# First three dense passes split over the columns of chunks 0 to 2 and chunk 3, and the check of w's range moved to GpSimd and ScalarE

## What is computed

```python
for t in range(S):
    cur = np.einsum('bhd,bhe->bhde', u[None] * kt, vt)
    y[:, :, t] = np.einsum('bhd,bhde->bhe', rt, state + cur)
    state = w[None, :, :, None] * state + np.einsum('bhd,bhe->bhde', kt, vt)
x = attention_out.transpose(0, 2, 1, 3).reshape(B * S, H * D)
x = (x @ w_a * (x @ w_b)) @ w_out
h = x @ w_in
out = (h * np.clip(h + 3.0, 0.0, 6.0) / 6.0) @ w_out2
```

## Time and profile before

| | |
|---|---|
| median of 3 runs | 919.12 us (918.99 to 919.4) |
| the profiled execution | 919.12 us |
| its span in the trace | 917.3 us |
| TensorE busy (PE) | 911.9 us |
| VectorE busy (DVE) | 369.5 us |
| ScalarE busy (ACT) | 329.5 us |
| GpSimd busy (POOL) | 184.3 us |

### The profile page before, as it was taken

One profiled execution on the slowest core, in us unless ns is written; L12 is line 12 of the kernel. 1 busy time (PEld: TensorE's weight loads), 2 busy tenths in 40 slices (PEclk: granted clock), 3 DMA queues, 4 the chain that ended last, 5 costly groups with the idle time before them and its releaser, 6 DMA issues.

```text
span 917.3 us, 15108 instructions
## 1 busy us (share of the span) xinstructions
PE 911.9 (99%) x6400; PEld 746.4 (81%) x6400; DVE 369.5 (40%) x607; ACT 329.5 (36%) x651; POOL 184.3 (20%) x168
## 2 busy tenths in 40 slices
PE   8999999999999999999999999999999999999998
PEld 6788888888888888888888888888888888888887
DVE  7746344525443343334222343343343343343332
ACT  6645323232333233242221343433333333333333
POOL 5976102111111111010755570000000000000000
PEclk9999999999999999999999999999999999999999
DMA  8653211121120121131311210100200100100000
GB/s 307 198 167 108 90 50 62 55 90 56 56 110 34 56 110 55 38 129 48 115 50 55 78 50 1 65 5 1 69 1 0 70 1 7 64 0 1 35 1 36
DMA packets 24281, 57.84 MB, mean 63 GB/s; under 512 B 2320, under 2 KB 8080, under 8 KB 24208
## 3 DMA queue, kind: packets, MB, share of 16 engines
q1 hardware_dynamic: 19808, 48.18, 15.6%
q10 hardware_dynamic: 4400, 8.65, 2.5%
HBM read 47.39 MB, written 9.44 MB: 62 GB/s over the span
## 4 chain that ended last, share of the span: by engine, by line
PE 98%; DVE 1%; DMA 0%; ACT 0%; issue 0%; SPq 0%; DVEq 0%; ACTq 0%
PE up_ps L722 32%; PE up_ps L799 21%; PE acc_ps L736 16%; PE acc_ps L813 11%; PE att_ps L813 11%; PE att_ps L614 2%; PE att_ps L677 1%; PE att_ps L682 1%; PE att_ps L646 1%; PE att_ps L663 1%; PE att_ps L671 1%; DMA first_rk<-in_rk_turned 0%; ACT A L854 0%; DVE first_rk L1044 0%; DVE first_A L1067 0%
## 5 line engine op out<-in xcount | busy, mean ns | idle before, releaser
L722 PE MATMUL up_ps<-x_cut,w_up 128*128 128x512 f32 x1296 | 307.3, 391 | 0.2 <-ACT x_cut L867 0.2
L722 PEld LDWEIGHTS up_ps<-x_cut,w_up 128*128 128x128 f32 x1296 | 241.7, 188 | 52.9 <-issue 3.0
L926 ACT ACTIVATE g_cut<-tmp 128x512 fp32r<-128x512 f32 x168 | 106.2, 632 | 214.4 <-DVE tmp L1149 141.6
L1157 DVE SCALAR_TENSOR_TENSOR g_cut<-tmp,g_cut 128x512 fp32r<-128x512 f32 x168 | 125.2, 745 | 117.5 <-ACT g_cut L926 117.5
L736 PE MATMUL acc_ps<-g_cut,w_down 128*128 128x512 f32 x648 | 157.3, 390 | 0.0
L736 PEld LDWEIGHTS acc_ps<-g_cut,w_down 128*128 128x128 f32 x648 | 121.3, 188 | 26.0 <-issue 0.6
L1151 DVE SCALAR_TENSOR_TENSOR tmp<-tmp,up_ps 128x512 f32<-128x512 f32 x96 | 66.1, 689 | 182.9 <-ACT tmp L920 182.9
L920 ACT ACTIVATE tmp<-up_ps,three 128x512 f32<-128x512 f32 x96 | 66.2, 690 | 171.0 <-PE up_ps L799 171.0
L1149 DVE TENSOR_TENSOR tmp<-tmp,up_ps 128x512 f32<-128x512 f32 x72 | 49.5, 688 | 169.7 <-PE up_ps L722 169.6
L799 PE MATMUL up_ps<-x_cut,w_up 128*128 128x512 f32 x432 | 105.7, 389 | 0.0
L799 PE MATMUL up_ps<-x_cut,w_in_first 128*128 128x512 f32 x432 | 105.4, 389 | 0.0
(11 more groups left out here) (109 smaller groups left out, 557.2 us busy)
## 6 DMA issues: line engine op xcount, KB each, us to landing
nat<-in_natural SPq DMA_DIRECT2D x20, 704.0 KB, 6.0
rkT<-in_rk_turned SPq DMA_DIRECT2D x20, 512.0 KB, 3.6
w_raw<-in_moe_w_out SPq DMA_DIRECT2D x28, 192.0 KB, 2.4
layer_out_T<-stage ACTq DMA_DIRECT2D x6, 768.0 KB, 3.4
x_cut<-layer_out_T SPq DMA_DIRECT2D x6, 768.0 KB, 4.3
outT<-stage ACTq DMA_DIRECT2D x5, 768.0 KB, 3.3
w_raw<-in_moe_w_in SPq DMA_DIRECT2D x12, 256.0 KB, 4.6
first_rk<-in_rk_turned SPq DMA_DIRECT2D x4, 512.0 KB, 5.6
```

The lines of the kernel that those rows point to most:

```text
L722: mm = pe.matmul(up_ps[:, m, :], w_up[i // PB][:, a, m, c, cols], x_cut[:, t % 2, b, c, :], start=(z == 0), stop=(z == len(order) - 1))
L926: nc.scalar.activation(g_cut[:, n % GR, HI, :], tmp[:, n % 2, :], ACT.Copy, scale=1.0 if n < TILES * N1 else 1.0 / 6.0).then_inc(s_gh, 1)
L1157: dve.scalar_tensor_tensor(out=lo, in0=tmp[:, n % 2, :], scalar=1.0 if n < TILES * N1 else 1.0 / 6.0, in1=hi.bitcast(F32), op0=ALU.mult, o ...
```

## The change

Five edits. The check of w moves from VectorE to GpSimd (`find_in_range`: two comparisons and a product, put between the fourth and the fifth of the eight masks that GpSimd makes), and the flag is made by one ScalarE instruction, Relu(count + `all_but_one`), straight from PSUM into the integer tile. The count goes into a bank of `att_ps`, not of `acc_ps`. TensorE now waits for three steps of `s_guard`. The dummy behind the count has 1 block, not 2. At the end of `first_chunks` the dummy of 1 block gives way to `first_passes`: the three high-by-high passes of the first `up1`, made over the 384 columns of chunks 0 to 2 as soon as those are there, and again over chunk 3's 128 columns. The first `up1` has six passes left.

```diff
+        def find_in_range(pool):
+            pool.wait_ge(s_w_u, 16)
+            nc.gpsimd.tensor_scalar(in_range[0:W2], w_col[0:W2], W_MIN, None, ALU.is_ge).then_inc(s_guard, 1)
+            nc.gpsimd.tensor_scalar(not_above[0:W2], w_col[0:W2], W_MAX, None, ALU.is_le).then_inc(s_guard, 1)
+            pool.wait_ge(s_guard, 2)
+            nc.gpsimd.tensor_tensor(out=in_range[0:W2], in0=in_range[0:W2], in1=not_above[0:W2],
+                                    op=ALU.mult).then_inc(s_guard, 1)
...
             keep_where(P + MID, every, 1, -1, 0, 1, ALU.is_equal)
+            find_in_range(pool)
             keep_where(2 * P, low_half, 1, -1, 0, 1, ALU.is_gt)
...
             if n == 0 and m == 0:
-                order.sort(key=lambda x: x[2])
+                order = sorted((x for x in order if x[1:] != (HI, HI)), key=lambda x: x[2])
             for z, (c, a, b) in enumerate(order):
-                if n == 0 and m == 0 and z == 2 * KC:
+                if n == 0 and m == 0 and z == KC:
                     pe.wait_ge(s_x_cut, B)
...
+        def first_passes(pe):
+            for chunks in (range(B - 1), range(B - 1, B)):
+                pe.wait_ge(s_x_high, chunks[-1] + 1)
+                if chunks[0] == 0:
+                    pe.wait_ge(s_w_high, KC)
+                cols = slice(chunks[0] * CH, (chunks[-1] + 1) * CH)
+                for c in range(KC):
+                    pe.matmul(up_ps[:, 0, cols], w_up[0][:, HI, 0, c, 0:P], x_cut[:, 0, HI, c, cols],
+                              start=(chunks[0] == 0 and c == 0), stop=False, skip_group_check=True)
...
             outputs(pe, 3)
-            keep_warm(pe, 1)
+            first_passes(pe)
...
-            dve.tensor_scalar(in_range[0:W2], w_col[0:W2], W_MIN, None, ALU.is_ge).then_inc(s_guard, 1)
-            dve.wait_ge(s_guard, 1)
-            dve.scalar_tensor_tensor(out=in_range[0:W2], in0=w_col[0:W2], scalar=W_MAX, in1=in_range[0:W2],
-                                     op0=ALU.is_le, op1=ALU.mult).then_inc(s_guard, 1)
...
-            dve.wait_ge(s_count, 1)
-            dve.tensor_scalar(all_in[:], count_ps, 3.0 * W2 * NP - 1.0, None, ALU.is_ge).then_inc(s_guard, 1)
-            dve.wait_ge(s_guard, 3)
-            dve.tensor_copy(flag[:], all_in[:]).then_inc(s_flag, 1)
...
                 nc.scalar.activation(first_use[:], three[:], ACT.Copy)
+                act.wait_ge(s_count, 1)
+                nc.scalar.activation(flag[:], count_ps, ACT.Relu, bias=all_but_one[:, 0:1]).then_inc(s_flag, 1)
                 flag_act = decide(act)
...
-                pe.wait_ge(s_guard, 2)
+                pe.wait_ge(s_guard, 3)
...
                 keep_warm(pe, 4)
-                keep_warm(pe, 2)
+                keep_warm(pe, 1)
                 first_chunks(pe)
```

More of the change, by code:

```diff
@@ L109, in build @@
             in_range = sb("in_range", [P, NP], of=setup)
-            all_in = sb("all_in", [1, 1], of=setup)
+            not_above = sb("not_above", [P, NP], of=setup)
+            all_but_one = sb("all_but_one", [1, 1], of=setup)
             inv_fine = sb("inv_fine", [P, NP, FINE + 1], of=setup)
@@ L306, in x_view @@
             return x_cut[:, tile % 2, z, :, cols_of(q)]
-        count_ps = acc_ps[0:1, 1, 0:1]
+        count_ps = att_ps[0:1, 0, 0:1]
         HD = H * D
@@ L722, in up1 @@
                 mm = pe.matmul(up_ps[:, m, :], w_up[i // PB][:, a, m, c, cols], x_cut[:, t % 2, b, c, :],
-                               start=(z == 0), stop=(z == len(order) - 1))
+                               start=(z == 0 and n + m > 0), stop=(z == len(order) - 1),
+                               skip_group_check=(n + m == 0))
             mm.then_inc(s_ua if m == 0 else s_ub, 1)
@@ L1182, in vector_layer2, with tables_of_powers @@
                         x2_low(dve, t + 1)
-        def guard_and_tables(dve):
+        def tables_of_powers(dve):
             links = [0]
@@ L1268, in _ @@
                 nc.gpsimd.memset(three[:], 3.0).then_inc(s_three, 1)
+                nc.gpsimd.memset(all_but_one[:], 1.0 - 3.0 * W2 * NP).then_inc(s_three, 1)
                 make_masks(pool)
@@ L1277, in _ @@
             def _(act):
-                act.wait_ge(s_three, 1)
+                act.wait_ge(s_three, 2)
                 nc.scalar.activation(first_use[:], three[:], ACT.Copy)
+                act.wait_ge(s_count, 1)
+                nc.scalar.activation(flag[:], count_ps, ACT.Relu, bias=all_but_one[:, 0:1]).then_inc(s_flag, 1)
                 flag_act = decide(act)
@@ L1301, in _ @@
             def _(dve):
-                guard_and_tables(dve)
+                tables_of_powers(dve)
                 flag_dve = decide(dve)
```

## The result

The changed kernel takes 921.76 us in the median of 9 runs (919.2 to 924.93); the kernel before took 919.4 us in the runs beside it (918.95 to 919.88). The ratio is 1.0033, with a 95% interval of 1.0023 to 1.0042: 0.33% slower. The forecast was 918.7 us and no difference. As telling as the median is the spread: 0.9 us before, 5.7 us after. One run took 919.2, the others form clumps at 921.1 to 921.8 and 923.8 to 924.9.

The account below looks back on a forecast made before the run. TensorE's queue from 20.55 us bounds the kernel, its start set by the front and the hand-over. 917.3 - 0.46 = 916.8 span, plus 1.8 around it, gives 918.66, forecast 918.7 us; range 918.1 to 919.5.

Parts of the forecast that it names:

- The check of w: Step on the start: `in_range` at 3.25 us, 0.28 later than before, covered by 0.3; taken as 0.
- 0.3 us of cover: Ahead of the own weights: 0.1 us of room behind the dummies plus about 0.2 from the halved dummy.
- TensorE's rate rises later: Rival, chance 0.06: gap ahead of the count and smaller dummy delay the rise past 7 us; 918.8 to 919.7.
- the 6.1 that the prediction named as a sign of being wrong: Sign at the start: prediction wrong if TensorE's own weights start later than 6.1 us; expected at 5.97.
- The hand-over: Stretch from 20.55 us to the transposes: they would start at 22.30, not 22.76, a gain of 0.46 us.
- The wide passes: Three 384-column passes in the last dummy's place: 0.63 us from 19.88, ending at 20.51, before the wait ends at 20.55.
- the narrow ones: Three 128-column passes behind chunk 3's high part: 0.34 us with the first load.
- the transposes' 0.08: Time taken for each narrow pass, from the spacing of four 112-column transposes with 128-column weight loads.
- the first load: Extra time of the first narrow pass at the hand-over, its weights loaded behind the wait: 0.10 us.
- The six full passes: Six 512-column passes left in the first `up1`, behind the narrow ones: 0.235 us each, 1.41 together.
- The rule that I set beside it: Skill's load cost at the hand-over: some 107 ns per 128 columns; narrow passes 0.32 instead of 0.24, gain 0.38.
- the margin at piece 19: Narrowest place found later on, piece 19's low part at 48.46 us: margin of 1.1 us shrinks to 0.65, stays open.

Follow-up runs that it names:

- the passes alone: Kernel before with `first_passes` in place of the last dummy and nothing else: 919.27 us, ratio 0.9999.
- the gap filled: Changed kernel plus one more dummy block ahead of the count, in the time TensorE waited for `in_range`: 918.95 us, then 918.97 us when timed again.

## Why the prediction was wrong, point by point

**The step that failed** is in "The check of w": the wait ahead of the count and the halved dummy were charged against 0.3 us of cover and put at 0. What they set off is the rival "TensorE's rate rises later": its mechanism was on the list, at a chance of 0.06 and with the wrong size. It named both causes, and the runs show each to be enough alone: 4 of 6 and 9 of 12 high with the gap, 8 of 12 with the block less, 0 of 11 and 1 of 12 with the gap filled. The price was put at up to 1 us (918.8 to 919.7), from one pair of dummies and one chunk's weights. Chunk 0's mask copy alone is 1.46 us late, and chunk 3's high part 5.35, because the half rate doesn't end with chunk 0: it lasted to some 19 us, and every chunk's own weights and weights are on the path while it does (VectorE and ScalarE, which set the pace before, wait for TensorE). In the two profiles of the levels between, at 921.71 and 920.61, the rise is at about 10 us.

**"Hidden, so nothing"** was the reasoning that let it pass. The gap and the shorter dummy were weighed as work that something else covers; but what the dummies do here, by the runs above, is to bring the rate up, and that was priced only as a rival. The Trainium skill ("TensorE: Matmul & The Clock Gate", section "What's actually happening") says that the engine's clock is throttled by default and activity lifts it, and that the moment isn't tied to the kernel's start. The traces agree, in that records take about twice their time until some moment that differs between executions with the same dummies (about 5.3 us in the profile of before, after 6.1 in that of the passes alone). The same page (section "Seeing it yourself") warns that the trace's own events of this clock have been unreliable. The granted clock here reads 1.00, the 2.4 GHz level, over stretches at half rate. That this half rate is the throttled clock is therefore argued, from the durations and from what sets it off, and no column here shows it.

**The check's lateness.** Forecast 3.25 us for `in_range`; it is 3.46. Each operation takes 0.20 to 0.24 us, as estimated, but they follow each other at 0.31, even the second, which waits for nothing. The count starts at 3.61 and not near 3.4, so the gap was 0.41 us where I had 0.3. The own weights start at 6.17 instead of 5.97: 0.2 late, which I had at 0, and above the 6.1 that the prediction named as a sign of being wrong.

**The hand-over.** Forecast 0.46 us, measured 0.37. The wide passes fit as forecast: they start at 25.24, and the narrow ones wait for chunk 3's high part and not for them. The three narrow weight loads stand from 25.91 to 26.32, 188 ns each, which spaces them by 0.11 us; I took the transposes' 0.08. The transposes were a poor stand-in: their weight loads are recorded at 138 to 143 ns, those of the narrow passes at 186 to 192. Yet the step from the first narrow load to the first full pass is 0.38, forecast 0.34, so that only about 0.05 of it is left for the first load, which I had at 0.10. The six full passes take 1.45 against 1.41, 0.04 more as well. Together that is the 0.09 by which the gain was overrated.

The rule that I set beside it (the Trainium skill, same page, section "LDWEIGHTS (loading the stationary operand)") is that a load costs by its columns, some 107 ns. The measured spacing of 0.11 us agrees. That its gain of 0.38 is also nearly the measured 0.37 is in part luck, since two smaller misses, the first load and the full passes, cancel.

**VectorE, ScalarE, SyncE.** The flag is there at 4.23 us instead of 4.47, the product starts at 5.05 instead of 5.23, since the transfer landed a little earlier in this execution. None of it shows in the time, as forecast. No new wait opened behind 22 us, so the margin at piece 19 held; the 0.6 us for `first_A` at 24.2 is the wait that stood at 18.9 before, with 0.5.

## What to carry to other kernels

Dummy matmuls that keep an engine busy are not slack, and a wait put ahead of them is not free even if nobody waits for their results. Where early records show the engine at half rate, price a shorter dummy or a new wait by what the work behind costs at that rate, over its whole length. Where the start of a kernel depends on such a rise, time enough runs to see levels; one profile, or three runs, can sit on either. And compare the duration of one known instruction at two times before believing a clock column.

## What the runs showed of the hardware

The half rate can last long into real work: from 6 to 19 us TensorE ran the chunks' small matmuls and short dummies, busy 9.01 of 9.01 us in one stretch by the profile, without coming up. Most times fell in levels some 2.7 to 2.9 us apart (919.1, 921.8, 924.7 with nine blocks). With ten or eleven blocks without a break 154 of 159 runs stayed below 920.5 us (the three groups of the kernel before and the six timings of such versions, the stray run left out), with nine or eight 8 of 24, with ten to twelve blocks and a gap 11 of 30. What exactly of TensorE's work decides it stays open: the runs tell amounts and gaps apart, but no version changed the shape of the dummies or their place in time alone.
